# One mixture-of-experts layer behind linear attention: the first layer of three experts on two thirds of the tokens by seven block products instead of eight

## The reference

```python
def _moe_ref(x, domain_probs, w1, w2):
    N, D = x.shape                 # 1536, 320
    E = w1.shape[0]                # 4 experts; w1 is 4x320x1024, w2 is 4x1024x320
    p = domain_probs / (domain_probs.sum(-1, keepdims=True) + 1e-09)
    out = np.zeros((N, D))
    for e in range(E):
        h = np.maximum(x @ w1[e], 0.0)
        out += p[:, e:e + 1] * (h @ w2[e])
    return out
```

## Time and profile before

| | |
|---|---|
| median of the runs | 419.06 us (417.49 to 419.07) |
| span of the profiled execution, first to last instruction | 416.4 us |
| device time of that execution | not recorded apart; the median is 2.7 us above the span |
| PE busy | 411.6 us, 99% |
| DVE, ACT, POOL busy | 180.6, 158.5, 152.3 us |
| granted TensorE clock | 1.000 over the span |

### The profile page before, as it was taken

How to read it: one execution, slowest core, us unless ns; L and a number is a source line. 1 busy time by engine, 2 the same in 40 slices (tenths; PEclk the granted TensorE clock), 3 DMA queues, 4 the chain that set the end, 5 groups by cost and what they waited for, 6 DMA issues and landing times.

```text
span 416.4 us, 7050 instructions
## 1 busy us (share of the span) xinstructions
PE 411.6 (99%) x2710; PEld 398.3 (96%) x2710; DVE 180.6 (43%) x372; ACT 158.5 (38%) x329; POOL 152.3 (37%) x189
## 2 busy tenths in 40 slices
PE   8999999999999999999999999999999999999997
PEld 8899999999999999999999999999999999999996
DVE  5875796646555556446223232323113132311313
ACT  4575477745355653514112431144211333211111
POOL 4865735595174925304011660065100453000000
PEclk9999999999999999999999999999999999999999
DMA  7999939678513845300000231024200000000101
GB/s 269 272 283 394 369 100 354 226 256 290 189 37 131 303 132 193 122 2 0 2 0 2 85 129 67 0 71 139 71 0 2 0 0 2 34 0 2 63 0 65
DMA packets 16899, 48.45 MB, mean 116 GB/s; under 512 B 1921, under 2 KB 8594, under 8 KB 15714
## 3 DMA queue, kind: packets, MB, share of 16 engines
q1 hardware_dynamic: 16290, 46.60, 31.9%
q10 hardware_dynamic: 576, 1.40, 1.0%
HBM read 45.94 MB, written 2.05 MB: 115 GB/s over the span
## 4 chain that ended last, share of the span: by engine, by line
PE 98%; DVE 1%; issue 0%; DVEq 0%
PE hid_ps L1076 42%; PE acc_ps L1095 37%; PE out_ps L1032 5%; PE score_ps L1095 3%; PE acc_ps L1076 2%; PE out_ps L1039 2%; PE score_ps L976 2%; PE add_ps L1011 1%; PE hid_ps L925 1%; PE score_ps L971 1%; PE acc_ps L1032 0%; PE out_ps L1051 0%; PE out_ps L1052 0%; PE out_ps L1053 0%; PE score_ps L989 0%
## 5 line engine op out<-in xcount | busy, mean ns | idle before, releaser
L810 DVE SCALAR_TENSOR_TENSOR h_lo<-hid_ps,h_hi 128x384 fp32r<-128x384 f32 (+2 forms) x120 | 68.0, 567 | 219.7 <-ACT h_hi L587 219.6
L587 ACT ACTIVATE h_hi<-hid_ps 128x384 fp32r<-128x384 f32 (+2 forms) x120 | 59.6, 497 | 231.9 <-PE hid_ps L1076 231.8
L1095 PE MATMUL acc_ps<-w_hi,h_hi 128*128 128x320 f32 x352 | 110.2, 313 | 0.0
L1095 PE MATMUL acc_ps<-w_hi,h_lo 128*128 128x320 f32 x352 | 108.8, 309 | 0.0
L1095 PE MATMUL acc_ps<-w_lo,h_hi 128*128 128x320 f32 x352 | 108.4, 308 | 0.0
L1076 PE MATMUL hid_ps<-xt_hi,w_hi 128*128 128x384 f32 (+2 forms) x360 | 104.1, 343 | 0.1
L1076 PE MATMUL hid_ps<-xt_hi,w_lo 128*128 128x384 f32 (+2 forms) x360 | 103.7, 342 | 0.0
L441 POOL TENSOR_TENSOR w_lo<-w_raw,w_hi 128x384 fp32r<-128x384 f32 x56 | 58.9, 1054 | 114.5 <-ACT w_hi L573 114.5
L1076 PEld LDWEIGHTS hid_ps<-xt_hi,w_lo 128*128 128x128 f32 x360 | 65.4, 189 | 4.3
L1095 PEld LDWEIGHTS acc_ps<-w_hi,h_hi 128*128 128x128 f32 x352 | 66.3, 188 | 1.3
L1095 PEld LDWEIGHTS acc_ps<-w_lo,h_hi 128*128 128x128 f32 x352 | 66.3, 188 | 1.3
(11 more groups left out here) (172 smaller groups left out, 371.9 us busy)
## 6 DMA issues: line engine op xcount, KB each, us to landing
w_raw<-in_w_b SPq DMA_DIRECT2D x27, 704.0 KB, 4.3
raw<-in_qk_s SPq DMA_DIRECT2D x8, 1024.0 KB
g_all<-g_dram SPq DMA_DIRECT2D x10, 512.0 KB, 6.1
kv<-in_kv_n SPq DMA_DIRECT2D x12, 352.0 KB, 5.9
q_pack<-in_q_p SPq DMA_DIRECT2D x10, 192.0 KB, 6.1
...
y_acc<-in_o_n SPq DMA_DIRECT2D x1, 1280.0 KB, 12.3
```

The source lines that it names most:

```text
L587: nc.scalar.activation(h_hi[:, M % RING, 0:cols], hid_bank(M)[:, 0:cols], ACT.Relu).then_inc(hid_hi, 1)
L810: nc.vector.scalar_tensor_tensor(h_lo[:, M % RING, 0:cols], hid_bank(M)[:, 0:cols], 0.0, h_hi[:, M % RING, 0:cols].bitcast(fp32), ALU.max, ...
L1095: last = nc.tensor.matmul(acc_ps[t][:, 0:DM], x, w, start=(f == 0 and i == 0), stop=(f == NF - 1 and i == 2))
```

## The change

The work of three experts (1, 2 and 0) on tiles 4 to 11 leaves the slots. What stays in slots: expert 0 on tiles 0 and 1, experts 1 and 2 on tiles 0 to 3 in pairs of tiles, expert 3 on all 12 tiles in threes, and expert 0 on tiles 2 and 3: 10 groups, 80 slots. Of these 48 slots have 2 tiles and 32 have 3.

The rest is done in 12 *steps* (3 experts, 4 steps each). A step covers two blocks of 128 hidden features and all 8 tiles, as two halves of 512 tokens. With the 320 input features cut in two halves of 160 this is a product of 2x2 by 2x2 blocks, and Strassen's scheme (in Winograd's form) needs seven block products for it in place of eight. Each is four matmuls of 512 columns: three for the 128 rows, and one of 96 rows in which high and low parts of the remaining 32 features are stacked. So a step has 28 such matmuls, where eight classical products would take 32. The second layer is as before: 48 matmuls of 320 columns per step (`wide_down`), for the step before or two before.

What is new beside the products: differences of the tokens' blocks, once (`make_whole`, `rest_whole`, `turn_whole`, `t_lows`, `rest_lows` on DVE; `turn_rest` on POOL; `round_rest`, `round_t` on ACT; 12 transfers inside SBUF in `load_rest`), sums of the weight blocks, once per step (`step_sums`, four on POOL), their splitting, and per step additions of the products (two products are kept in SBUF by ACT, four additions lie on DVE, one on POOL) before the relu. The first product of step 0 stands behind `down(76)`, the next three behind slots 77, 78 and 79. The last two units make no additions, weighed keys and state. T0, CAST, SUB and EARLY are moved to the new groups. Sequences that the rows below show are left out of this cut diff.

```diff
-LOADS = (0, 1, 2, 3, 2, 1, 0)
-GROUPS = ((0, 0, 2), (1, 0, 2), (1, 2, 2), (2, 0, 3), (2, 3, 3), (3, 0, 3), (3, 3, 3), (3, 6, 3), (3, 9, 3),
-          (4, 6, 3), (4, 9, 3), (5, 4, 4), (5, 8, 4), (6, 10, 2), (6, 2, 4), (6, 6, 4))
+LOADS = (0, 1, 2, 3, 0)
+GROUPS = ((0, 0, 2), (1, 0, 2), (1, 2, 2), (2, 0, 2), (2, 2, 2), (3, 0, 3), (3, 3, 3), (3, 6, 3), (3, 9, 3), (4, 2, 2))
...
-T0 = {2: 2, 3: 6, 4: 16, 5: 22, 6: 28, 7: 32, 8: 38, 9: 44, 10: 48, 11: 54}
-EARLY = 24
+T0 = {2: 2, 3: 6, 4: 16, 5: 22, 6: 29, 7: 35, 8: 41, 9: 46, 10: 51, 11: 56}
+EARLY = 36
...
+EXPERTS = (1, 2, 0)
+STEPS = len(EXPERTS) * NF // 2
+REM = 3 * 32
+SUM_AT = 2 * DM + 4 * 256
+W_STEP = SUM_AT + 4 * 256
+ORDER = (1, 6, 5, 7, 2, 4, 3)
...
+BEGIN = 76
+W_RING = 4
...
+def halves_of(t):
+    first, second = ((0, t - 1), (1, t - 2)) if t % 2 == 0 else ((1, t - 2), (0, t - 1))
+    return [(half, p) if 0 <= p < STEPS else None for half, p in (first, second)]
...
+            def load_step(q):
+                if q < 2:
+                    sp.wait_ge(w_lo_done, N_BLOCKS - 4 * (1 - q))
+                else:
+                    sp.wait_ge(own_low, q - 1)
+                    sp.wait_ge(s_rest_low, q - 1)
+                    sp.wait_ge(s_down_low, q - 1)
+                sp.dma_start(step_raw(q)[:, 0:SUM_AT], w_s[q]).then_inc(s_in[q % 2], 16)
...
+                if M == T0[NT - 1] + 7:
+                    load_rest()
+                if M == 70:
+                    load_step(0)
+                if M == 74:
+                    load_step(1)
...
+            def turn_rest():
+                pool.wait_ge(rest_ready, 2)
+                i_1, i_2, j_2, j_1 = (rest_hi[:, n, :] for n in range(4))
+                nc.gpsimd.tensor_tensor(rest_t[:, 0, :], j_1, i_1, ALU.subtract).then_inc(rest_t_ready, 1)
+                nc.gpsimd.tensor_tensor(rest_t[:, 2, :], j_2, j_1, ALU.subtract).then_inc(rest_t_ready, 1)
...
+            def step_sums(q):
+                pool.wait_ge(s_in[q % 2], 16 * (q // 2 + 1))
+                wait_if(pool, sums_high, q - 1)
+                a_21, a_11, a_12, a_22, s_1, s_2, s_3, s_4 = (step_blocks(q, n, 1) for n in range(8))
...
+                nc.gpsimd.tensor_tensor(s_4, a_12, s_2, ALU.subtract).then_inc(sums_ready, 1)
+            def own_lows(q):
+                pool.wait_ge(own_high, q + 1)
+                raws = step_blocks(q, 1, 3).rearrange("p (o c) -> p o c", o=3)
+                nc.gpsimd.tensor_tensor(left_lo(q, 0, 3), raws[:, :, 0:128], left_hi(q, 0, 3)[:, :, 0:128].bitcast(fp32),
+                                        ALU.subtract).then_inc(own_low, 1)
...
                     count_weights(k)
-                    weigh_keys(k)
+                    if k < NT - B:
+                        weigh_keys(k)
                 if (k := unit_at(M, 2)) is not None:
                     scale_q(k)
-                if (k := unit_at(M, 6)) is not None:
+                if (k := unit_at(M, 6)) is not None and k < NT - B:
                     carry_state(k)
                 for w in blocks_to_split(M):
                     split_low(w)
+                if M == 67:
+                    turn_rest()
+                if M == 73:
+                    step_sums(0)
+                if M == 75:
+                    own_lows(0)
+                if M == 76:
+                    step_sums(1)
+                if M == 78:
+                    step_down_low(0)
+            own_lows(1)
+            step_down_low(1)
+            add_22(0)
+            for t in range(1, STEPS):
+                if t + 1 < STEPS:
+                    step_sums(t + 1)
+                    own_lows(t + 1)
+                    step_down_low(t + 1)
+                add_22(t)
...
+            def own_highs(q):
+                act.wait_ge(s_in[q % 2], 16 * (q // 2 + 1))
+                if q < 2:
+                    act.wait_ge(down_done, (75, 78)[q])
...
+                nc.scalar.activation(left_hi(q, 0, 3), step_blocks(q, 1, 3).rearrange("p (o c) -> p o c", o=3), ACT.Copy)\
+                    .then_inc(own_high, 1)
+            def sums_highs(q):
+                act.wait_ge(sums_ready, 4 * q + 4)
+                nc.scalar.activation(left_hi(q, 3, 4), step_blocks(q, 4, 4).rearrange("p (o c) -> p o c", o=4), ACT.Copy)\
+                    .then_inc(sums_high, 1)
...
+                if M == 68:
+                    round_rest(0, 3)
+                if M == 70:
+                    round_t(0)
+                if M == 71:
+                    round_t(2)
+                if M == 72:
+                    round_rest(3, 2)
+                if M == 73:
+                    round_rest(5, 2)
+                if M == 75:
+                    own_highs(0)
+                    sums_highs(0)
+                if M == 77:
+                    keep_1(0)
+                if M == 78:
+                    step_down_high(0)
...
+                if M == 79:
+                    keep_5(0)
+            sums_highs(1)
+            step_down_high(1)
...
+                if t > 0:
+                    keep_1(t)
+                    if t + 1 < STEPS:
+                        own_highs(t + 1)
+                    keep_5(t)
...
+                        step_down_high(t + 1)
+                        sums_highs(t + 1)
+                wide_relu(t, 11)
...
+            def turn_whole(which):
+                x_11, x_12 = whole[:, 0, 0:WIDE], whole[:, 0, WIDE:]
+                x_21, x_22 = whole[:, 1, 0:WIDE], whole[:, 1, WIDE:]
+                if which == 0:
+                    dve.wait_ge(whole_ready, 2)
+                    nc.vector.tensor_tensor(whole_t[:, 0, :], x_12, x_11, ALU.subtract).then_inc(t_ready, 1)
+                    nc.vector.tensor_tensor(whole_t[:, 2, :], x_22, x_12, ALU.subtract).then_inc(t_ready, 1)
...
+            def t_lows(first):
+                dve.wait_ge(t_high, first // 2 + 1)
+                nc.vector.tensor_tensor(t_lo[:, first:first + 2, :], whole_t[:, first:first + 2, :],
+                                        t_hi[:, first:first + 2, :].bitcast(fp32), ALU.subtract).then_inc(t_low, 1)
...
+            def sums_lows(q):
+                dve.wait_ge(sums_high, q + 1)
+                raws = step_blocks(q, 4, 4).rearrange("p (o c) -> p o c", o=4)
+                nc.vector.tensor_tensor(left_lo(q, 3, 4), raws[:, :, 0:128], left_hi(q, 3, 4)[:, :, 0:128].bitcast(fp32),
+                                        ALU.subtract).then_inc(sums_low, 1)
+            def step_rest_low(q):
+                dve.wait_ge(own_high, q + 1)
+                dve.wait_ge(sums_high, q + 1)
+                raws = step_blocks(q, 1, 7).rearrange("p (o c) -> p o c", o=7)[32:64, :, 128:256]
+                low = left_hi(q)[32:64, :, 128:256]
+                nc.vector.tensor_tensor(low, raws, low.bitcast(fp32), ALU.subtract).then_inc(s_rest_low, 1)
...
                         split_down_low(w)
+                if M in (64, 65):
+                    make_whole(M - 64)
+                if M in (66, 67):
+                    rest_whole(2 * (M - 66))
+                if M in (68, 69, 70):
+                    turn_whole(M - 68)
+                if M in (71, 72):
+                    t_lows(2 * (M - 71))
+                if M == 73:
+                    rest_lows(0, 3, 0)
+                if M == 74:
+                    rest_lows(3, 2, 1)
+                if M == 75:
+                    rest_lows(5, 2, 2)
+                if M == 76:
+                    sums_lows(0)
+                    step_rest_low(0)
+                if M == 78:
+                    add_2(0)
+            add_3(0)
+            sums_lows(1)
...
+            def product(t, m):
+                bank = wide_bank[m]
+                if m == 1:
+                    pe.wait_ge(own_low, t + 1)
+                    pe.wait_ge(s_rest_low, t + 1)
+                    if t == 0:
+                        pe.wait_ge(t_low, 2)
+                        pe.wait_ge(rest_low, 3)
+                        pe.wait_ge(p_ready, 2 * NT)
+                        pe.wait_ge(fresh_ready, NT - B)
...
+                if right < 3:
+                    x_hi, x_lo = (x[:, min(right, 1), wide_tok[right // 2]] for x in (xt_hi, xt_lo))
+                else:
+                    x_hi, x_lo = t_hi[:, right - 3, :], t_lo[:, right - 3, :]
+                nc.tensor.matmul(bank[:, :], hi[:, 0:128], x_hi, start=m in (1, 5, 6), stop=False, skip_group_check=True)
+                nc.tensor.matmul(bank[:, :], lo, x_hi, start=False, stop=False, skip_group_check=True)
+                nc.tensor.matmul(bank[:, :], hi[:, 0:128], x_lo, start=False, stop=False, skip_group_check=True)
+                nc.tensor.matmul(bank[:, :], hi[0:REM, 128:256], rest[:, right, :], start=False, stop=True, skip_group_check=True)\
+                    .then_inc(product_done, 1)
+            def wide_down(half, p, i):
+                if i == 0:
+                    pe.wait_ge(low_of[11 + half], p + 1)
...
+                        pe.wait_ge(acc_free, wide_evictions(p, half, i) - 4)
```

(23 more changed lines are left out.)

288 lines of the change are left out of this document (272 added, 16 removed).

## The result

The changed kernel takes 438.19 us (median of 4 runs, 436.85 to 440.59) against 419.06: ratio 1.0485, 95% interval 1.0462 to 1.0508, slower by 19 us. Forecast were 431.5 us, with 415 to 438 as the range, so the time lies 0.2 us above the range and 6.7 above the forecast. The profiled execution took 436.85 us, 435.1 of them in the span.

What follows compares the result with a forecast made beforehand. The kernel was taken to be as long as PE's list. Span: 416.4 - 12.3 (list) + 16.2 (preparation) + 6.5 (first steps) + 1 + 1 (rhythm, slots 34 to 41) = 428.8 us; with 2.7 more, 431.5, range 415 to 438.

Steps and rivals of the forecast that it cites:

- PE's list: Whole kernel: PE's matmul work gets 12.3 us shorter, 11.1 from fewer products and 1.2 from two units without additions.
- Slots 34 to 41: Attention slots, some shortened to 1.84 us: POOL's splits meet unit 7, `scale_q(7)` a little late; 1 us, bounds 0 and 4.
- The preparation: Slots 66 to 76: POOL and DVE not ready for the first product, 16.2 us late; bounds 5.5 and 18.
- the prediction's own sign: Wrong if the first product waits below 6 us, POOL's and DVE's SBUF operations overlap at usual times, or PE's list lacks 12.3.
- The predicted mechanism: Preparation: POOL's and DVE's SBUF operations exclude each other for whole instructions, so both queues add up to 33.6 us.
- The first two steps: Expert part's start: chains have less cover, so products of step 1 and step 2 wait; 6.5 us, bounds 3 and 10.
- The step's rhythm: All steps: the handoff before the first `wide_down` of every second step slightly late; 1 us in all, bounds 0 and 6.
- The 2.7 between span and time: Whole kernel: the median of the runs taken as 2.7 us above the span.
- Rival 3: PE cools down in its pause before the first product and runs at half speed: 5.5 us more, 437; chance 0.14.
- rival 1: Everything is covered: PE stays dense and the first product starts at its turn, 406.8 us; chance 0.13.
- rival 2: Preparation and first steps: POOL and DVE hold each other up less, some operations slip through, 417.2 us; chance 0.13.

Runs made afterwards that it cites:

- experiment 1: The kernel before with only the changed attention plan (groups, start slots, casts, subtractions), no Strassen product: 429.24 us, ratio 1.0249.
- experiment 6: Strassen products for two experts only, with the attention plan of the kernel before: 423.56 us; with unread filler matmuls before the first products of steps 1 and 2, 423.46.
- experiment 3: Changed kernel with POOL waiting for DVE before its last four splits: 440.4 us; without `rest_lows`: 441.53; without `rest_lows` and POOL waiting before two splits: 436.85.
- experiment 7: Changed kernel with POOL's waits and unit 7's start and subtractions moved: 437.22 us; also first product two slots later: 432.31; later product with two Strassen experts: 420.41.
- experiment 8: Step 1's roundings and low parts, and later `step_rest_low`, earlier, on kernels with first product two slots later: two Strassen experts 415.04 us, three (unit 7, POOL's waits changed) 430.12.
- experiments 4: Changed kernel with unread filler matmuls in PE's four long waits, before `down(73)` and the first products of steps 0 to 2: 438.37 us, ratio 1.0476.

## Why the prediction came out as it did

The direction held. One term of the sum, the attention's, was sized far too small, and it makes the difference; the largest term, the preparation's, came out near its size by another path than the one predicted.

- *PE's list, -12.3.* Steady steps are 13.5 us, slots 1.84 and 2.73 as priced, and 434.7 of the 435.1 us of span follow with it. Right.
- *Slots 34 to 41, 1 us (bounds 0 and 4).* This is the step that failed: the term was 8.2 us too small. I looked for trouble only where POOL's splits meet unit 7. The plan packs units 5 to 11 into shorter slots all the way from 24 to 56, and there it lost 9.2 us in the profiled execution, where the sum had 1; alone the plan costs 10.7 us in the time, 8.0 in the execution that kept full clock (experiment 1). The splits were one cause, as I had them (`q_pack` late twice, 2.2 us); the larger part of the waits was DVE's order, which I had not walked: a subtraction directly ahead of the scores that need it, behind `gate_x` (3.0), or ahead of `add_expert` (1.6). Only 3.2 us were moved by new tables, and these did not show in the time; the rest was not taken apart further, except that before's own plan loses none of it (experiment 6). Whether other start slots could save the new plan is not shown.
- *The preparation, +16.2.* The prediction counts from `up(73)` (its slot 66, at -15.9, is `up(67)` at 218.68), which started at 234.59. So the first product came 23.7 us behind that point for 25.4 predicted, and 14.5 us late for 16.2. That it is so near is in part luck. Predicted were two queues that take turns until the sums are there at 21.6, and 3.8 us behind them. In the changed kernel the sums were there at 16.4: the pairs of splits followed each other every 1.76 us for 1.88, DVE got nothing until POOL's row was nearly through, and two of the three `rest_lows` (2.4 us) stood behind the sums. Then 7.3 us followed, not 3.8. The chain of the trace goes from `t_lows(0)` to the low part of slot 73, into four blocks of PE that took 6.0 us for 3.7, at a granted clock of 0.52, and only then to ACT's roundings. So by the prediction's own sign it was wrong here: the first product waited 2.5 us, below the 6 it named, POOL's splits kept their times but for the first two of the row, and the wait of 9.3 us stood at `down(73)`. The predicted mechanism is the limit once DVE is let in (experiment 3): the sums then end 18.7 us behind `up(73)`, and 4.3 us less work gives 3.3. And even then it is no lower bound for PE's loss: two slots of classical work moved ahead of the first product gave 4.9 us back (experiment 7), and that choice was nowhere in the prediction.
- *The first two steps, +6.5.* From the first product to that of step 3 PE lost 7.1 us, 1.6 of them before the second product; right within its bounds. Waits are 4.3 of it (2.1, 0.2, 1.4 and 0.6), the rest blocks that took longer than their list. It was order for the greater part: experiment 8 takes 5.4 us off with two experts, 2.2 with three.
- *The step's rhythm, +1.* Measured 0. With the terms above, 8.2 more, 1.7 less, 0.6 more and 1 less, that makes 6.1 of the 6.3 us by which the span of 435.1 exceeds the 428.8 of the sum. The 2.7 between span and time were 3.1.
- *Rival 3, the clock.* It did fall, and the blocks behind the waits took up to twice their time, 1.77 us for 0.88. The sum had nothing for it, and in the trace it cost something on the way to the second product: 2.3 us on the chain behind `down(73)` and 1.6 behind the first product. With fillers the first product came 10.7 us behind PE's restart, not 11.4. But the medians show no gain from them (experiments 4 and 6; the intervals are 2 and 1 us to either side). Its mechanism was right, its price of 5.5 us no run shows.
- *Rivals 1 and 2.* The first product started 14.5 us behind its turn, so rival 1 fell; `t_lows(0)` did not slip through between POOL's operations but stood still for 9 us, so rival 2 did too. Covered work does exist, but with two experts and a new order, not here.

What stays open: the time of the changed kernel lies 1.3 us above its profiled execution, and its executions are 3.7 us apart where before's are 1.6. Traces of the same instructions differ in three things: the clock, below; `t_lows(0)`, 10.5 us here and 11.9 to 12.1 in five others; and waits of 0.2 to 0.6 us for low parts of weights before 40 us. Which of the executions had them can't be said for those without a trace.
